# Gate values through a matrix product instead of a DRAM round trip, and the gather queue as loops

## The reference

```python
x = attention(q, k, v)                      # 4 batches x 768 rows -> x is 3072 x 512
# first mixture: top 1 of 8 experts
logits = x @ w_gate;  e = argmax(logits)
gate_w = softmax(logits)[e]
eom = 1 / (1 + exp(-(x @ w_output_gate)))   # 3072 x 8
y[mask_e] = gate_w * eom[:, e] * (relu(x[mask_e] @ w1[e]) @ w2[e])   # 512 -> 1024 -> 512
# second mixture on y: 3072 / 8 = 384 tokens for each expert, highest logits first
out[mask_e] = relu(y[mask_e] @ w21[e]) @ w22[e]
```

## Time and profile before

| | |
|---|---|
| median of three runs | 1041.1 us |
| the profiled execution | 1037.06 us |
| its span, first to last instruction | 1035.1 us |
| PE, DVE, ACT, POOL busy | 88%, 65%, 44%, 22% of the span |
| attention and logits | up to about 244 us |
| first routing | 244 to 262 us |
| blocks of the first mixture | 262 to 634 us |
| second routing | 634 to 745 us |
| second mixture | 745 us to the end |

### The profile page before, as it was taken

The page is one execution under the profiler, slowest core; times in us unless marked ns, Lnnn a source line. Parts: engine busy times, 40 slices in busy tenths (PEclk is TensorE's granted clock), DMA queues, the critical chain, the costliest instruction groups (busy, mean ns, idle before and its releaser), DMA issues.

```text
span 1035.1 us, 22030 instructions
## 1 busy us (share of the span) xinstructions
PE 911.7 (88%) x6375; PEld 765.8 (74%) x6376; DVE 676.0 (65%) x1812; ACT 450.6 (44%) x983; POOL 226.1 (22%) x247
## 2 busy tenths in 40 slices
PE   6889999894899999999999984444599999999996
PEld 3777777782688888888888873333398989898985
DVE  5677888777666867969878685555554645454431
ACT  3678888856525253544525250000042434343410
POOL 2222322300322222223222221000203222322211
PEclk8899999996999999999999996555699999999999
DMA  9567767352352433516334251000136354544200
GB/s 216 108 160 163 168 161 170 93 189 84 126 201 71 172 115 139 203 41 205 134 117 166 80 192 58 2 2 2 36 109 209 127 174 161 190 144 164 90 31 30
DMA packets 147597, 129.43 MB, mean 125 GB/s; under 512 B 103468, under 2 KB 115780, under 8 KB 147396
## 3 DMA queue, kind: packets, MB, share of 16 engines
q1 hardware_dynamic: 137696, 99.68, 32.4%
q0 software_dynamic: 9792, 28.86, 8.1%
q10 hardware_dynamic: 36, 0.01, 0.0%
HBM read 107.81 MB, written 20.72 MB: 124 GB/s over the span
## 4 chain that ended last, share of the span: by engine, by line
PE 71%; DVE 10%; issue 6%; SPq 6%; DMA 3%; DVEq 2%; ACT 1%; POOL 0%; ACTq 0%; POOLq 0%
PE ps_s L1282 15%; PE ps_o L1305 14%; PE ps_o L1658 9%; PE ps_s L1642 6%; PE ps_pT L1642 6%; PE ps_s L1658 4%; DMA qn<-in_q 3%; PE ps_t L1819 3%; PE ps_pT L1293 2%; PE ps_o L518 2%; SPq L2071 2%; SPq L2090 2%; DVE product L1497 1%; PE ps_t L1268 1%; PE ps_t L471 1%
## 5 line engine op out<-in xcount | busy, mean ns | idle before, releaser
L1305 PE MATMUL ps_o<-w_split_parts,hs 128*128 x696 | 168.4, 398 | 6.7 <-issue 6.7
L1282 PE MATMUL ps_s<-w_split_parts,xs 128*128 x696 | 165.9, 394 | 2.3 <-ACT xs L1375 1.4
L1305 PEld LDWEIGHTS ps_o<-w_split_parts,hs 128*128 128x128 f32 x696 | 130.0, 190 | 33.9 <-issue 7.2
L1497 DVE SCALAR_TENSOR_TENSOR product<-y_sb,wg_all 128x512 bf16<-128x512 f32 x224 | 145.8, 689 | 10.6 <-issue 5.8
L1282 PEld LDWEIGHTS ps_s<-w_split_parts,xs 128*128 128x128 f32 x696 | 128.6, 188 | 28.3 <-issue 2.8
L834 ACT ACTIVATE arena_p<-arena_p,min_s 128x256 f32<-128x256 f32 (+1 forms) x192 | 92.3, 484 | 28.4 <-DVE min_s L699 27.8
L1658 PE MATMUL ps_o<-w_split_parts,hs 128*128 128x512 f32 x384 | 94.6, 398 | 0.0
L1488 DVE TENSOR_TENSOR w_split_parts<-raw,w_split_parts 128x1024 f32 (+1 forms) x68 | 78.7, 1221 | 19.4 <-ACT w_split_parts L1394 18.1
L1658 PEld LDWEIGHTS ps_o<-w_split_parts,hs 128*128 128x128 f32 x384 | 70.2, 188 | 16.5 <-ACT hs L1692 2.9
L1738 DVE TENSOR_TENSOR w_split_parts<-raw,w_split_parts 128x1024 fp32r<-128x1024 f32 x56 | 68.6, 1225 | 19.8 <-ACT w_split_parts L1700 19.7
L1570 POOL DMA_INDIRECT xg<-x_rows,rows_i x31 | 42.5, 1372 | 173.1 <-issue 157.6
(11 more groups left out here) (312 smaller groups left out, 1681.5 us busy)
## 6 DMA issues: line engine op xcount, KB each, us to landing
raw<-in_moe_w SPq DMA_DIRECT2D x32, 2048.0 KB, 9.4
y_rows<-y_sb POOLq DMA_DIRECT2D x31, 256.0 KB, 2.3
kn<-in_k SPq DMA_DIRECT2D x32, 192.0 KB, 3.5
qn<-in_q SPq DMA_DIRECT2D x32, 192.0 KB, 3.7
vn<-in_v SPq DMA_DIRECT2D x32, 192.0 KB, 2.9
x_rows<-arena_x SPq DMA_DIRECT2D x96, 64.0 KB, 1.6
va<-in_v SPq DMA_DIRECT2D x32, 120.0 KB, 2.7
wg_rows<-in_moe_w_gate SPq DMA_DIRECT2D x1, 2048.0 KB, 7.6
```

The costliest lines, as they stand in the source:

```text
L1282: last = nc.tensor.matmul(ps_s[:, f, :], xs[:, a, c * P:(c + 1) * P], weights(par, w, cols), start=(n == 0), stop=(n == len(passes) - 1))
L1305: last = nc.tensor.matmul(ps_o[:, 0, :], hs[:, a, c * P:(c + 1) * P], weights(par, 2 + w, slice(c * DM, (c + 1) * DM)), start=(n == 0), st ...
L1497: nc.vector.scalar_tensor_tensor(product[:, e % 2, :], y_sb[:], 1.0, wg_all[:, e, :], ALU.mult, ALU.mult, accum_out=log_now[:, e:e + 1])
```

## The change

The DRAM buffer of the gate values, their transpose, copy, store and the 31 gathers are taken out. Instead the gate values pass through a second table like that of the token numbers. DVE cuts each value into three bf16 parts that add up to it, multiplies them with the block's one-hot matrix (three more `dve_vals`, with three sets instead of two: 93 columns), PE adds up 24 more products into a bank of `ps_o`, and DVE adds the three parts into `gates`. ACT waits once for `gates_known`, before its first `high_h`. POOL's program becomes three loops; as an index in a loop has to be in a register, each gather after the first copies its column of `rows_i` into `row_now` first.

```diff
-            nc.vector.tensor_tensor(gate[:, 0:C], t2[:, 0:C], m_open[:, 0:C], ALU.mult).then_inc(gate_made, 1)
+            done(nc.vector.tensor_tensor(gate[:, 0:C], t2[:, 0:C], m_open[:, 0:C], ALU.mult))
+            for part in range(3):
+                done(nc.vector.tensor_copy(gate_parts[:, part, 0:C], gate[:, 0:C]))
+                if part < 2:
+                    done(nc.vector.tensor_tensor(gate[:, 0:C], gate[:, 0:C], gate_parts[:, part, 0:C], ALU.subtract))
+        def dve_gate_table(dve):
+            for part in chunks(TILES):
+                dve_vals(part, 3, BLK1, gate_parts).then_inc(row_hots, 1)
+        def dve_gates(dve):
+            dve.wait_ge(tabled, 2)
+            high, mid, low = [ps_o[:, 1, part * BLK1:(part + 1) * BLK1] for part in range(3)]
+            nc.vector.tensor_copy(gates[:], low)
+            dve.drain()
+            nc.vector.tensor_tensor(gates[:], gates[:], mid, ALU.add)
+            dve.drain()
+            nc.vector.tensor_tensor(gates[:], gates[:], high, ALU.add).then_inc(gates_known, 1)
...
-            act.wait_ge(gate_turned, 1)
-            nc.scalar.activation(gate_rows, ps_s[0:TILES, 2, 0:P], ACT.Copy).then_inc(gate_copied, 1)
-            act.wait_ge(gate_copied, 1)
-            act.dma_start(gate_dram.rearrange("(c p) o -> c (p o)", p=P), gate_rows).then_inc(gate_stored, 16)
...
-            pe.wait_ge(gate_made, 1)
-            nc.tensor.transpose(ps_s[0:TILES, 2, 0:P], gate[:, 0:TILES], ident[:]).then_inc(gate_turned, 1)
             turn_x(0)
             up(0)
             turn_x(1)
+            pe_table(pe, ps_o[:, 1, :], len(chunks(TILES)), TILES, 3, BLK1)
             turn_h(0)
...
-                act.wait_ge(gate_in, b * 16 + 16)
...
             high_x(1)
+            act.wait_ge(gates_known, 1)
             begin(0)
-            act.wait_ge(gate_stored, 16)
...
                 low_x(0)
+                dve_gate_table(dve)
                 low_w(0, 0, 1, range(4), n=0)
                 low_x(1)
                 return
+            dve_gates(dve)
             low_h(0)
...
-                if b > 0:
+                rows = rows_i
+                if not (isinstance(b, int) and b == 0):
                     pool.wait_ge(gathered, b * 16)
                     pool.wait_ge(x_turned, b)
+                    rows = row_now
+                    nc.gpsimd.tensor_copy(row_now[:], rows_i[:, bass.ds(b, 1)]).then_inc(row_copied, 1)
+                    pool.wait_ge(row_copied, b)
                     apart(pool)
...
-            for b in range(BLK1 + 3):
-                if b < BLK1:
-                    gather(b)
-                if 1 <= b < BLK1 + 1:
-                    gather_gate(b - 1)
-                if b >= 3:
-                    put(b - 3)
+            gather(0)
+            with pool.Fori(1, 3) as b:
+                gather(b)
+            with pool.Fori(3, BLK1) as b:
+                gather(b)
+                put(b - 3)
+            with pool.Fori(BLK1 - 3, BLK1) as b:
+                put(b)
```

More of the change, by code:

```diff
@@ L60, in program @@
     y_dram = nc.dram_tensor("y_rows", (BLK1 * P, DM), f32).ap()
-    gate_dram = nc.dram_tensor("gate_rows", (NT, 1), f32).ap()
     q_p, k_p, v_p = [t.rearrange("b (g a) (i r) d -> (b g) a r i d", a=2, r=P) for t in (q, k, v)]
@@ L110, in program @@
         slot_parts = sb("slot_parts", [P, 4, COLS], bf16)
+        gate_parts = sb("gate_parts", [P, 3, COLS], bf16)
         row_no = sb("row_no", [P, P, PART], bf16)
@@ L185, in program @@
         NE = BLK1 * E
-        NV = 4 * BLK2 * COLS
+        NV = max(3 * BLK1, 4 * BLK2) * COLS
         (lg_, lw_, t3_, one_hot_, chosen_, cum_, above_, equal_, ge_, m, m_open, t2, t2b, left, taken, hi, lo, pos,
@@ L199, in program @@
             t[:] for t in (bucket, code_now, code_all, span, scale, diag, most_2)]
-        gate_rows = t3_[0:TILES, 0:P]
         lg, lw, t3 = grid(lg_, BLK1, 2 * E), grid(lw_, BLK1, E), grid(t3_, BLK1, E)
@@ L216, in program @@
         dest_i = sb("dest_i", [P, BLK2], i32)
+        row_now = sb("row_now", [P, 1], i32)
         rows2_now = sb("rows2_now", [P, CB], i32)
@@ L293, in program @@
         blocks_known = sem("blocks_known")
-        gate_made = sem("gate_made")
-        gate_turned = sem("gate_turned")
-        gate_copied = sem("gate_copied")
-        gate_stored = sem("gate_stored")
-        gate_in = sem("gate_in")
+        gates_known = sem("gates_known")
         slow_tables = sem("slow_tables")
@@ L302, in program @@
         rise_open = sem("rise_open")
+        row_copied = sem("row_copied")
         gathered = sem("gathered")
@@ L1564, in gather @@
             def gather(b):
-                if b > 0:
+                rows = rows_i
+                if not (isinstance(b, int) and b == 0):
                     pool.wait_ge(gathered, b * 16)
                     pool.wait_ge(x_turned, b)
+                    rows = row_now
+                    nc.gpsimd.tensor_copy(row_now[:], rows_i[:, bass.ds(b, 1)]).then_inc(row_copied, 1)
+                    pool.wait_ge(row_copied, b)
                     apart(pool)
                 nc.gpsimd.indirect_dma_start(out=xg[:], out_offset=None, in_=x_dram[:, :],
-                                             in_offset=bass.IndirectOffsetOnAxis(rows_i[:, b:b + 1], 0),
+                                             in_offset=bass.IndirectOffsetOnAxis(rows[:, 0:1], 0),
                                              bounds_check=NT - 1, oob_is_err=False).then_inc(gathered, 16)
-            def gather_gate(b):
-                if b == 0:
-                    pool.wait_ge(gate_stored, 16)
-                else:
-                    pool.wait_ge(gate_in, b * 16)
-                nc.gpsimd.indirect_dma_start(out=gates[:, b:b + 1], out_offset=None, in_=gate_dram[:, :],
-                                             in_offset=bass.IndirectOffsetOnAxis(rows_i[:, b:b + 1], 0),
-                                             bounds_check=NT - 1, oob_is_err=False).then_inc(gate_in, 16)
             def put(b):
                 pool.wait_ge(scaled, b + 1)
-                pool.dma_start(y_out[b], y_sb[:]).then_inc(y_put, 16)
-            for b in range(BLK1 + 3):
-                if b < BLK1:
-                    gather(b)
-                if 1 <= b < BLK1 + 1:
-                    gather_gate(b - 1)
-                if b >= 3:
-                    put(b - 3)
+                pool.dma_start(y_out[bass.ds(b, 1)].rearrange("a r d -> (a r) d"), y_sb[:]).then_inc(y_put, 16)
+            gather(0)
[6 more added lines that the diff above has]
+                put(b)
             pool.wait_ge(y_put, BLK1 * 16)
@@ L1802, in program @@
         PHASES = E - 1
-        HOT_CHUNKS = len(chunks(TILES))
+        HOT_CHUNKS = len(chunks(TILES)) * 2
         def pe_routing2(pe):
@@ L2041, in dve_routing2 @@
             dve_positions(dve, 2, C, BLK2, True, slot_parts)
-            dve.wait_ge(tabled, 2)
+            dve.wait_ge(tabled, 3)
             tables_of(tables)
@@ L2057, in dve_routing2 @@
                 dve_positions(dve, 3, C, BLK2, True, slot_parts, False)
-                dve.wait_ge(tabled, 3)
+                dve.wait_ge(tabled, 4)
                 tables_of(slow_tables)
```

## The result

The changed kernel takes 1046.07 us (median of 5 runs, 1045.14 to 1048.16), the kernel before 1041.1 in the same runs; the ratio is 1.0065, 95% interval 1.0046 to 1.0085. So it is slower by 5 to 9 us. The prediction was no change, 1040.8 with a range from 1035.5 to 1046. The profiled execution took 1046.24 us, of which 1044.5 are its span, against 1035.1 before: 9.3 more (1044.46 for 1035.12).

A forecast was written before the change was run, and what follows sets the result against it. PE was taken to bound the loop at 12.2 us a block. Terms −0.6 + 2.0 − 0.95 gave +0.45 at `turn_x(2)`, −0.33 at `down_(0)` after the gather's rule, carried through: 1040.8 us on the median, range 1035.5 to 1046.

The forecast's parts named there:

- Step 7: Behind the blocks: nothing changes but where the code lies; a jump's 3.30 us there is left as it was.
- Step 2: PE behind `turn_x(1)`: the table's 24 products of 93 columns add 2.0 us, ends 1.7 and 4.3.
- Step 1: Start of the blocks: without turn, copy and store, ACT's `high_x(0)` starts 0.6 us earlier (0.7 to 0.3).
- Step 3: PE ahead of `up(1)`: the gap of 0.95 us goes, as loads run beside the table; other end 0.
- Step 4: Third gather: released 0.6 us earlier, copy and wait add 0.25; its landing puts `down_(0)` at 279.15, not 279.48.
- Step 5: ACT's wait for `gates_known`: DVE's jump ends at 276.3, gate values at 277.0, `down_(0)` covered by 1.0 us; cost 0.
- Step 6: In the loop, on POOL: each gather of rows comes 0.25 us later, with 1.66 free; cost 0.
- POOL's loops: Rival: POOL idles at each backward jump, each gather comes 3.30 or 4.92 us later; +10 to +20 us; chance 0.07.
- the stalls behind jumps: Rival: DVE's 3.30 us and other stalls behind jumps shrink with the code's new place; −3 to −6 us; chance 0.1.
- the second rival: Start of the blocks: PE's table dear (+2.3 us) or DVE's gate values late (+3.9); median 1043 to 1045; chance 0.2.
- the faster rival: Stalls behind jumps, DVE's 3.30 us and a few others, shrink with the code's place; −3 to −6 us; chance 0.1.

The follow-up runs named there:

- `table_only`: The changed kernel with GpSimd's queue written out for all blocks, without loops or copies of the rows' column; ratio 1.0078 to the kernel before.
- `loops_only`: The kernel before with GpSimd's queue as loops, rows and gate values through copied columns, gate values still through DRAM; ratio 1.0012.
- `after_late`: The changed kernel with one GpSimd drain added in the last expert of the second mixture, where GpSimd idles; ratio 0.9966 to the kernel before.
- `before_again`: The kernel before, unchanged, profiled a second time; span 1036.4 us.
- `after_drain`: The changed kernel with one GpSimd drain added behind the first mixture's last put; ratio 1.0023 to the kernel before, median 1041.89 us.

## Why the prediction was wrong

Step 7 failed first: "Behind the blocks nothing changes but where the code lies." The change takes 31 DMAs off GpSimd's queue, and with that the program's last drain grows from 4.49 to 9.07 us: +4.6, half of the 9.3 us between the two profiled executions and two thirds of the 6.8 that the ratio gives. It is in every profile, goes with the gathers and not with the loops (`table_only`, `loops_only`), and vanishes when the drain is hidden: by the two ratios `after_late` is 1% under the changed kernel. Why 31 DMAs fewer make it longer, when each adds to it, is the clearing that the kernel before gets and the changed one doesn't. I had looked for what waits for the gathers and for nothing that comes of having issued them; the 6.7 us from the last issue to the end of the span could be seen before.

Step 2 failed by its size. 24 products took 4.09 us, not 2.0. The end that I gave as "if the price doesn't follow the clock", 4.3, was the true case: I halved the price of a row at half clock, where the reads of the moving operand set it. With 4.09 for 2.0 the turn and no longer the gather decides at `down_(0)`, and the sum would have been +1.6 there (−0.6 + 4.09 − 0.95 − 0.91). The Trainium skill (Advanced Engine Details and Errata, "SBUF Cachelines") says that reads which go to another line of 16 B each time pay a penalty. By it a penalty was due, as the elements lie 64 B apart; of the clock, and so of the halving, it says nothing. The trace agrees for the moving operand (0.042 us contiguous, 0.159 with 64 B) and less for the stationary one (0.063); that 80 B cost more than 64 it doesn't say.

The fall of the clock behind the table had no term. It cost some 1.3 us in the profiled execution (18.11 for 16.80), and not in each one.

Step 1 was right in kind: ACT began 0.84 us earlier, of which 0.5 was gained before the first table already, so some 0.35 of the 0.6. Step 3 was right: the gap ahead of `up(1)` is gone. Step 4's queue was right (0.88 us between copy and gather, as in the earlier trace rows), its place of decision wrong: the turn came later than the landing, so `down_(0)` waited for nothing and its gap went whole. The copy took 0.18 us at the third gather, so the up to 1.3 us that the prediction held possible there didn't come; a copy of 0.93 us, beside VectorE's instructions of 1.2 us on the weights, did occur at the next gather, which had time. Step 5 was right: jump 4.42 for 4.92, gate values at 276.3, covered; the cover was larger since PE was later. Step 6 was right: the loop costs nothing.

Of the rivals, POOL's loops fell (ratio 1.0012 with them alone), and the stalls behind jumps stayed: 3.20 us for the 3.30 of the earlier trace rows. Of the second rival, at a chance of 0.2, the dear table came true and the late gate values didn't; the table alone would have ended within 0.5%. That the time came out beside the range's upper end, which was this rival's sum, is luck: most of it is the drain, which no rival had. Two of the prediction's figures also don't follow from its words: the lowest run less the smaller part of the faster rival (1037.06 − 3) is 1034.1 and not 1035.5, and a table of 4.3 us adds 2.2 and not 2.3 to its sum. Neither changes the outcome.

Behind `down_(0)` TensorE loses another 2.6 us between the two profiled executions, and nothing here shows it to be more than chance. 1.6 of it lies in the first 24 products of the second mixture, 5.99 us for 4.40, where a low clock lasted longer, and `before_again` has 5.99 too. TensorE's last product ends at 1025.8 to 1030.3 us in the seven profiles without the table (mean 1028.5), and at 1028.0 to 1031.8 (mean 1029.8) in the changed kernel, `table_only`, `after_drain` and `after_late`: 1.3 us later in the mean, close to the table's net price, though the ranges overlap.

Sum by the parts that repeat: 4.6 for the drain, 1.4 to 2.8 for the table, −0.3 for step 1, together 5.7 to 7.1, against a measured 5 to 9.

Not settled: what shortens GpSimd's list by itself, at which DMA and by how many; what decides whether the clock falls behind the table. Whether the table is worth anything once the drain is hidden can't be told: 0.9966 with it, 0.9947 to 0.9978 without.

## What to carry to other kernels

Look at the time from the last transfer's landing to the end of the span. If GpSimd issues DMAs, its last drain may lie there. It grows with them (0.082 us each here), and one `drain` put where GpSimd idles takes it off the end. Before scaling a product's price with the clock, ask whether its moving operand is contiguous; and before making it so, ask what the engine that writes it will pay.

## What the runs showed of the hardware

- GpSimd's drain: 0.06 us + 0.082 us for each DMA issued since the last drain, gathers, scatters and plain puts alike, long after they had landed, at 3 to 110 DMAs. Lists of 125 to 141 DMAs, all with small ones among them, had 58 or 87 cleared without a drain, in the kernel before somewhere from the 94th to the 138th.
- A bf16 product of 93 columns: 0.042 us with contiguous operands at full clock, 0.079 at half; 0.063 with 64 B between the stationary operand's elements; 0.159 with 64 B between moving elements at either clock; with the stationary operand strided too 0.170, and 0.192 at 80 B in both.
- VectorE: 744 bf16 results written 186 B apart took 3.53 us, 0.54 in runs of eight side by side; 1024 compared with a value held along the inner axis 1.22, with one that changes along it 0.69.
